# Two order changes at the start of a retention, mixer and MLP kernel: the output decays are loaded ahead of the first chunk's values, and the first chunk's x is finished ahead of its state

## The chip, the cores and the metric

The kernel runs on one core of a Trainium2 chip, in one launch. The metric is the device time of the launch in microseconds (us). The engines are named as in the profile: PE is TensorE (matmul; PEld its weight loads), DVE is VectorE, ACT is ScalarE, POOL is GpSimd, SP is SyncE. Each runs its own stream of instructions in order, and waits for the others only at semaphores. Transfers (DMA) are issued from SP's, ACT's and POOL's queues.

## The reference

Three stages follow each other on two batches of 768 tokens with 512 features (8 heads of 64):

```python
# 1: retention, a decayed running state per head
for t in range(S):
    state = gamma[None, :, None, None] * state + einsum('bhd,bhe->bhde', k[:, :, t], v[:, :, t])
    y[:, :, t] = scale * einsum('bhd,bhde->bhe', q[:, :, t], state)
# 2: x = y as (B, S, 512); a wave-like mixer over tokens, then a channel layer
theta = x @ w_theta
y = einsum('ts,bsd->btd', w_tok_r, x * cos(theta)) + einsum('ts,bsd->btd', w_tok_i, x * sin(theta))
u = x + y
x = u + maximum(u @ w_ch, 0)
# 3: a two-layer mixer over tokens, a two-layer MLP over channels, both with a residual
u = x + (maximum(x^T @ w_tok1, 0) @ w_tok2)^T
out = u + maximum(u @ w_ch1, 0) @ w_ch2
```

The change lies wholly in the first 13 us of stage 1, and only the first of its chunks is touched.

## The kernel before

**Tiling of stage 1.** Each batch's 768 tokens are cut into 6 chunks of 128, so there are 12 chunks, g = 0 to 11. Retention is computed a chunk at a time: the part within the chunk as a masked product of queries and keys, the part from earlier chunks through a state. The decays are constant factors, held in the tile `cst`: the first part (triangle, score, key and carry decays, identity) is loaded by ACT's queue under the semaphore `const_in`, the last part, `out_decay` (C_OUT to N_CONST, 128 x 512 floats, 256 KB), by SP's queue under `decay_in`.

**One chunk's steps**, by the names of the functions and the lines of the profile:

- SP loads q, k (transposed), k and v (by rows) of the chunk into `qkv_in` (L380, 1 MB). Chunk 0 is loaded in two halves: L394 (q and k transposed, semaphore `first_qk_in`) and L395 (k and v by rows, the "values", semaphore `chunk_in[0]`). L396 loads the output decays.
- PE `scores(g)` (L999): queries times keys, 16 matmul records.
- DVE `weigh(g)` (L712): scores times the causal decays, into `prob`.
- PE `outputs(g)` (L1029, from the state, not for the first chunk of a batch; L1039, from `prob` and v), into the banks BK_Y.
- POOL `decay_keys(g)` (L439): k by rows times the key decays, into `k_dec`.
- PE `keys_values(g)` (L1013): the chunk's own contribution to the state, into BK_STATE.
- DVE `advance_state(g)` (L722 for the first chunk of a batch, L725 otherwise): BK_STATE into `state`.
- DVE `finish_x(g)` (L731): BK_Y times `out_decay`, into `res`. This is x of the chunk.
- ACT `x_high(g)` (L553) and DVE `x_low(g)` (L736): x as a pair of rounded parts, for products at higher precision. `theta_high` (ACT, L536) and `theta_low` (DVE, L696, twice) make the same pair of w_theta, once.
- PE `theta(g)` (L982): x times w_theta, 12 matmuls. It waits for `x_lo_ready` and, for the first chunk, `theta_lo`.
- After that come angles, sines and cosines on ACT and DVE, and PE's `turn_x(g)` (L1053).

**What sets the order.** It is written out by hand, engine by engine. PE's order at the start is: two rounds of idle matmuls (L988), scores(0), outputs(0), keys_values(0), scores(1), keys_values(1), outputs(1), theta(0), scores(2), keys_values(2), outputs(2), and so on. DVE's order is: a memset, the causal decays (L809), weigh(0), a wait for `decay_in`, and then for each g advance_state(g), finish_x(g), weigh(g+1), x_low(g); after x_low(0) come the two theta_low. ACT's is x_high(0), then the two theta_high. SP's is the two halves of chunk 0, the output decays, chunk 1, the two halves of w_theta, chunk 2 and so on.

The waits around the change: outputs(1) waits for `x_ready` of finish_x(0), because it writes the banks BK_Y that finish_x(0) reads. keys_values(1) waits for `state_ready` of advance_state(0). SP's load of chunk 3 waits for outputs(0) and keys_values(0) on PE. Nothing else waits for `decay_in` but the DVE.

The quoted functions hold the order of DVE at the start and that of SP's loads.

Of the kernel before, what the change touches and what calls it, by code (L numbers as in the profile page):

```python
# [13 lines left out]
NG = B * NC  # L14
# [72 lines left out]
C_OUT = C_IDENT + P  # L87
N_CONST = C_OUT + DM
# [16 lines left out]
def retention_mixer_mlp(nc, qkv, theta_w, tok, weights, ch2, consts, out):  # L105
    with ExitStack() as ctx:
        def sb(name, shape, dt=F32, within=ctx):
            return within.enter_context(nc.sbuf_tensor(name, shape, dt))

        def sem(name):  # L110
            return ctx.enter_context(nc.semaphore(name))

        cst = sb("cst", [P, N_CONST])
# [108 lines left out]
        def res_half(b, k, half):  # L222
            return res[:, b, k, half * HS:(half + 1) * HS]
# [11 lines left out]
        def parts_of(b, n):  # L235

            return sum(tile in (b, 2) for _, tile in HIDDEN[:n])
# [10 lines left out]
        decay_in = sem("decay_in")  # L248
# [84 lines left out]
        def split_done(eng, i):  # L333
            if i < MIDDLE:
                eng.wait_ge(middle_lo, i + 1)
            else:
                eng.wait_ge(late_lo, i - MIDDLE + 1)
# [35 lines left out]
        @block.sync  # L373
        def _(sp):
            def load_chunk(g):
                if g >= NQ:
                    sp.wait_ge(y_ready, g - NQ + 1)
                if g == NQ:
                    sp.wait_ge(kv_ready, 1)
                sp.dma_start(qkv_in[:, g % NQ, :], qkv[g]).then_inc(chunk_in[g % NQ], 16)  # L380

            def load_piece(i):
                if i >= NSTAGE:
                    split_done(sp, i - NSTAGE)
                sp.dma_start(stage[:, i % NSTAGE, :], weights[i]).then_inc(piece_in[i % NSTAGE], 16)

            def load_third(e):

                q, at = (2, 1, 0)[1 + e // 3], slice(e % 3 * THIRD, (e % 3 + 1) * THIRD)
                if e == 3:  # L390
                    sp.wait_ge(theta_lo, 2)
                sp.dma_start(raw[:, q, at], tok[2 * q, :, at]).then_inc(third_in[e], 16)

            sp.dma_start(qkv_in[:, 0, 0:2 * DM], qkv[0, :, 0:2 * DM]).then_inc(first_qk_in, 16)  # L394
            sp.dma_start(qkv_in[:, 0, 2 * DM:4 * DM], qkv[0, :, 2 * DM:4 * DM]).then_inc(chunk_in[0], 16)  # L395
            sp.dma_start(cst[:, C_OUT:N_CONST], consts[:, C_OUT:N_CONST]).then_inc(decay_in, 16)  # L396
            load_chunk(1)
            for i in range(2):
                at = slice(i * THETA_HALF, (i + 1) * THETA_HALF)
                sp.dma_start(raw[:, 0, at], theta_w[:, at]).then_inc(theta_in[i], 16)  # L400
            for g in range(2, NG):
                load_chunk(g)
                if g < 8:
                    load_third(g - 2)

            sp.wait_ge(zr_ready, NG)
            sp.wait_ge(zi_ready, NG)
            for i in range(N_PIECES):
                load_piece(i)

            split_done(sp, N_PIECES - 1)
            for i in range(2):
                sp.dma_start(w2_raw[:, i, :], ch2[i]).then_inc(w2_in[i], 16)
            for p, r, b in ((1, 0, 0), (4, 1, 0), (5, 1, 1), (6, 0, 1)):
                for i in range(CELLS):
                    m, half = i // 2, i % 2
                    sp.wait_ge(down_kept, p * CELLS + i + 1)
                    sp.dma_start(out[b, 2 * r + m, :, half * HS:(half + 1) * HS],
                                 res_half(b, 2 * r + m, half)).then_inc(out_sent, 16)
            sp.wait_ge(out_sent, 16 * 4 * CELLS)  # L420
# [271 lines left out]
        def _(dve):  # L692
            def theta_low(i):
                at = slice(i * THETA_HALF, (i + 1) * THETA_HALF)
                dve.wait_ge(theta_hi, i + 1)
                dve.scalar_tensor_tensor(out=w_sq[:, 1, at], in0=raw[:, 0, at], scalar=TURNS, in1=f32(w_sq[:, 0, at]),  # L696
                                         op0=ALU.mult, op1=ALU.subtract).then_inc(theta_lo, 1)

            def token_low(p, third):
                at = slice(third * THIRD, (third + 1) * THIRD)  # L700
                dve.wait_ge(tok_hi, 3 * (p if p > 1 else 1 - p) + third + 1)
                dve.tensor_tensor(tw[:, p % 2, 1, at], raw[:, W_RAW[p], at], f32(tw[:, p % 2, 0, at]),  # L702
                                  ALU.subtract).then_inc(tok_lo, 1)
# [6 lines left out]
            def weigh(g):  # L710
                dve.wait_ge(score_ready, g + 1)
                dve.tensor_tensor(prob[:, :, :], ps[:, BK_SCORE:BK_SCORE + 2, :], causal[:, :, :],  # L712
                                  ALU.mult).then_inc(prob_ready, 1)

            def advance_state(g):
                b, c = g // NC, g % NC
                if c == NC - 1:
                    return
                dve.wait_ge(kv_ready, b * (NC - 1) + c + 1)
                new, kv = state[:, (g + 1) % 2, :], ps[:, BK_STATE, 0:H * D // 2]  # L720
                if c == 0:
                    dve.tensor_scalar(new, kv, 1.0, None, ALU.mult).then_inc(state_ready, 1)  # L722
                else:
                    dve.wait_ge(carried_ready, b * (NC - 2) + c)
                    dve.tensor_tensor(new, kv, carried[:, :], ALU.add).then_inc(state_ready, 1)  # L725

            def finish_x(g):
                dve.wait_ge(y_ready, g + 1)
                to = res[:, g // NC, :, g % NC * P:(g % NC + 1) * P].rearrange("p (r m) t -> p r m t", r=2)
                y = ps[:, BK_Y:BK_Y + 2, 0:2 * P].rearrange("p r (m t) -> p r m t", m=2)  # L730
                dve.tensor_tensor(to, y, out_decay.rearrange("p r (m t) -> p r m t", m=2),  # L731
                                  ALU.mult).then_inc(x_ready, 1)

            def x_low(g):
                dve.wait_ge(x_hi_ready, g + 1)
                dve.tensor_tensor(x_lo[:, g % 2, :, :], res[:, g // NC, :, g % NC * P:(g % NC + 1) * P],  # L736
                                  f32(x_hi[:, g % 2, :, :]), ALU.subtract).then_inc(x_lo_ready, 1)

            def reduce_angle(g):
                t = turn[:, g % 2, :]  # L740
                dve.wait_ge(whole_ready, g + 1)
                if g >= 2:
                    dve.wait_ge(zi_ready, g - 1)

                dve.scalar_tensor_tensor(out=t, in0=fold[:, g % 2, :], scalar=-ROUND, in1=bank(BK_THETA + g % 2),
                                         op0=ALU.add, op1=ALU.subtract).then_inc(frac_ready, 1)
                dve.wait_ge(frac_ready, g + 1)
                dve.tensor_scalar(t, t, 0.5, -0.5, ALU.min, ALU.max).then_inc(angle_ready, 1)
# [13 lines left out]
            def z_low(s):  # L762
                p, i = s // NPAIR, s % NPAIR
                dve.wait_ge(z_hi, s + 1)
                what, hi, lo = z[:, Z_KIND[p], i, :], zs[:, s % NZ, 0, :], zs[:, s % NZ, 1, :]
                if Z_SIGN[p] > 0:
                    dve.tensor_tensor(lo, what, f32(hi), ALU.subtract).then_inc(z_lo, 1)
                else:
                    dve.scalar_tensor_tensor(out=lo, in0=what, scalar=-1.0, in1=f32(hi), op0=ALU.mult,
                                             op1=ALU.subtract).then_inc(z_lo, 1)  # L770
# [43 lines left out]
            for g in range(NG + 2):  # L814
                if 0 <= g - 2:
                    reduce_angle(g - 2)
                if g < NG:
                    advance_state(g)
                    finish_x(g)
                if g + 1 < NG:  # L820
                    weigh(g + 1)
                if g < NG:
                    x_low(g)
                if g == 0:
                    for i in range(2):
                        theta_low(i)
                if g >= NG - 1:
                    z_low(g - (NG - 1))
                if g >= 2:
                    turn_parts(g - 2)  # L830
                    if g < 8:
                        token_low(1 - (g - 2) // 3, (g - 2) % 3)
# [450 lines left out]
```

## Time and profile before

| | |
|---|---|
| median of 3 runs | 435.82 us (435.68 to 436.22) |
| the profiled execution | 435.77 us, of which the span from first to last instruction 434.0 us |
| PE busy | 426.8 us, 98% of the span |
| DVE busy | 278.4 us, 64% |
| ACT busy | 158.3 us, 36% |
| POOL busy | 85.3 us, 20% |
| granted TensorE clock | 0.999 of full speed on average |
| the chain that ended last | PE 96%, DVE 2%, DMA 1% of the span |

Busy shares say how much of the span an engine had an instruction in work. The chain that ended last is followed back from the last instruction, at each step to what released it. Every microsecond outside PE in it is a place where PE had to wait. PE is busy in 98% of the span, so all that PE waits for is a few microseconds, most of them in the first 15. A time in a row of the timeline is the start in us from the span's start and then the duration; the end is their sum. On one engine, neighbouring instructions overlap by a little where neither waits.

### The profile page before, as it was taken

The numbers are of one execution on the slowest core, as the hardware profiler recorded it, in microseconds if no ns is written. First come the engines' busy times: TensorE is split into PE (matmuls) and PEld (weight loads), VectorE is DVE, ScalarE is ACT, GpSimd is POOL, SyncE is SP. The second block draws the span as 40 slices with busy tenths as digits, with TensorE's granted clock in tenths as the row PEclk, the third lists the DMA queues.
The fourth block names the chain that finished last, engine by engine and source line by source line (L and its number), as shares of the span: only waits on it lengthen the run. The fifth ranks groups of instructions, "written<-read, shape, count | busy, mean of one in ns | idle before, by whom it ended". The sixth has DMA issues, their size and how long they took to land.

```text
span 434.0 us, 6621 instructions
## 1 busy us (share of the span) xinstructions
PE 426.8 (98%) x2748; PEld 388.3 (89%) x2748; DVE 278.4 (64%) x383; ACT 158.3 (36%) x231; POOL 85.3 (20%) x75
## 2 busy tenths in 40 slices
PE   7999999999999999999999999999999999999997
PEld 4778878899999999999889988888888899999997
DVE  3799998799999995234415304525211599999951
ACT  1364564744455456112214311101202443555500
POOL 1322241000300006980005803303000110000000
PEclk9999999999999999999999999999999999999999
DMA  8975797540594102030000000003000468340121
GB/s 301 419 269 198 253 270 146 103 145 2 157 220 159 48 2 97 2 115 31 0 2 0 2 0 0 2 0 142 5 0 2 72 154 171 113 67 26 54 74 73
DMA packets 10478, 42.25 MB, mean 97 GB/s; under 512 B 1104, under 2 KB 3280, under 8 KB 8656
## 3 DMA queue, kind: packets, MB, share of 16 engines
q1 hardware_dynamic: 7344, 26.74, 16.6%
q0 software_dynamic: 2960, 14.94, 15.6%
q8 instruction: 22, 0.36, 0.4%
q10 hardware_dynamic: 144, 0.14, 0.1%
q14 instruction: 8, 0.07, 0.1%
HBM read 38.68 MB, written 3.15 MB: 96 GB/s over the span
## 4 chain that ended last, share of the span: by engine, by line
PE 96%; DVE 2%; DMA 1%; ACT 0%; issue 0%; ACTq 0%; DVEq 0%
PE ps L982 85%; PE ps L999 3%; PE ps L1039 3%; PE ps L1053 2%; PE ps L1130 1%; PE ps L1013 1%; PE ps L1029 1%; DMA qkv_in<-qkv 1%; DVE prob L712 1%; DVE h_ops_c L906 0%; DVE w_sq L696 0%; ACT h_ops_c L657 0%; DVE x_lo L736 0%; DVE res L731 0%; DVE res L942 0%
## 5 line engine op out<-in xcount | busy, mean ns | idle before, releaser
L982 PE MATMUL ps<-u,ch 128*128 128x512 f32 x432 | 98.1, 389 | 0.0
L982 PEld LDWEIGHTS ps<-u,ch 128*128 128x128 f32 x432 | 81.1, 188 | 16.8
L982 PE MATMUL ps<-tw,zs 128*128 128x384 f32 x504 | 88.1, 335 | 0.0
L982 PEld LDWEIGHTS ps<-tw,zs 128*128 128x128 f32 x504 | 87.3, 188 | 0.1
L982 PE MATMUL ps<-h_ops_c,w 128*128 128x384 f32 x312 | 57.0, 335 | 0.2
L982 PEld LDWEIGHTS ps<-h_ops_c,w 128*128 128x128 f32 x312 | 54.2, 188 | 0.8 <-DVE h_ops_c L906 0.8
L899 DVE SCALAR_TENSOR_TENSOR h_a<-ps,h_a 128x512 f32<-128x512 f32 (+1 forms) x16 | 8.9, 558 | 44.3 <-PE ps L982 26.3
L580 ACT ACTIVATE zs<-z 128x768 fp32r<-128x768 f32 x28 | 23.7, 846 | 37.0 <-PE ps L982 37.0
L982 PE MATMUL ps<-ut,w_sq 128*128 128x384 f32 x192 | 35.5, 338 | 0.0
L982 PEld LDWEIGHTS ps<-ut,w_sq 128*128 128x128 f32 x192 | 33.0, 188 | 0.0
L982 PE MATMUL ps<-w_sq,x_hi 128*128 128x512 f32 x96 | 30.7, 401 | 0.7 <-DVE w_sq L696 0.7
L642 ACT ACTIVATE h_a<-ps 128x512 f32<-128x512 f32 (+1 forms) x16 | 7.9, 491 | 54.2 <-PE ps L982 54.2
L982 PE MATMUL ps<-h_ops_a,w 128*128 128x384 f32 x144 | 27.6, 334 | 0.0
L982 PEld LDWEIGHTS ps<-h_ops_a,w 128*128 128x128 f32 x144 | 25.2, 188 | 0.1
L454 POOL TENSOR_TENSOR ut<-res,ut 128x384 fp32r<-128x384 f32 x16 | 16.6, 1076 | 33.0 <-ACT ut L585 33.0
L460 POOL TENSOR_TENSOR u<-res,u 128x768 fp32r<-128x768 f32 x8 | 14.7, 1843 | 40.2 <-ACT u L636 40.2
L667 ACT ACTIVATE w<-w_raw 128x1536 fp32r<-128x1536 f32 x7 | 10.4, 1486 | 32.0 <-PE ps L982 32.0
L553 ACT ACTIVATE x_hi<-res 128x512 fp32r<-128x512 f32 x12 | 7.6, 633 | 39.2 <-DVE res L731 39.2
L982 PEld LDWEIGHTS ps<-w_sq,x_hi 128*128 128x128 f32 x96 | 17.2, 188 | 4.0 <-issue 0.9
L849 DVE SCALAR_TENSOR_TENSOR res<-ps,res 128x384 f32<-128x384 f32 x16 | 8.9, 558 | 18.3 <-PE ps L982 18.3
L702 DVE TENSOR_TENSOR tw<-raw,tw 128x768 fp32r<-128x768 f32 x21 | 20.7, 984 | 0.0
L626 ACT ACTIVATE u<-ps 128x512 fp32r<-128x512 f32 x12 | 7.2, 600 | 34.2 <-PE ps L1130 34.2
(106 smaller groups left out, 639.0 us busy)
## 6 DMA issues: line engine op xcount, KB each, us to landing
qkv_in<-qkv SPq DMA_DIRECT2D x11, 1024.0 KB, 7.5
raw<-tok POOLq DMA_DIRECT2D x7, 1152.0 KB, 9.0
stage<-weights SPq DMA_DIRECT2D x11, 512.0 KB, 3.4
w_raw<-ch POOLq DMA_DIRECT2D x7, 768.0 KB, 6.8
cols_out<-res SPq DMA_DIRECT2D x16, 192.0 KB, 1.8
raw<-tok SPq DMA_DIRECT2D x6, 384.0 KB, 8.6
w_raw<-ch SPq DMA_DIRECT2D x2, 768.0 KB, 5.3
raw<-tok POOLq DMA_DIRECT2D x3, 384.0 KB, 9.2
```

The costliest lines, as they stand in the source:

```text
L454: pool.tensor_tensor(u_half(1, b, k, half), res_half(b, k, half), f32(u_half(0, b, k, half)), ALU.subtract).then_inc(ut_lo, 1)
L460: pool.tensor_tensor(u[:, b, 1, k, :], res[:, b, k, :], f32(u[:, b, 0, k, :]), ALU.subtract).then_inc(u2_lo, 1)
L580: act.activation(zs[:, s % NZ, 0, :], z[:, Z_KIND[p], i, :], ACT.Copy, scale=Z_SIGN[p]).then_inc(z_hi, 1)
L642: act.activation(hidden_units(f % 2, f // 2, 0)[:, cols], bank(BK_H2[n % 8])[:, 0:cols.stop - cols.start], ACT.Relu).then_inc(h2_first, 1)
L667: act.activation(w2[:, p % 2, 0, :], w2_raw[:, W2_RAW[p], :], ACT.Copy, scale=W2_SIGN[p]).then_inc(w2_hi, 1)
L702: dve.tensor_tensor(tw[:, p % 2, 1, at], raw[:, W_RAW[p], at], f32(tw[:, p % 2, 0, at]), ALU.subtract).then_inc(tok_lo, 1)
L849: dve.scalar_tensor_tensor(out=part, in0=ps[:, BK_M + q % 2, 0:HS], scalar=0.0, in1=part, op0=ALU.max, op1=ALU.add).then_inc(x2_kept, 1)
L899: dve.scalar_tensor_tensor(out=hidden_units(half, phi, 1)[:, cols], in0=bank(BK_H2[n % 8])[:, at:at + cols.stop - cols.start], scalar=0.0, ...
L982: mm = pe.matmul(dst, left(l), right(r), start=first and n == 0, stop=last and n == 2, skip_group_check=True)
L999: mm = pe.matmul(ps[:, BK_SCORE + r, i * P:(i + 1) * P], qkv_in[rows, g % NQ, DM + i * P:DM + (i + 1) * P], qkv_in[rows, g % NQ, i * P:(i ...
L1039: mm = pe.matmul(ps[cols, BK_Y + r, i // 2 * P:(i // 2 + 1) * P], qkv_in[:, g % NQ, 3 * DM + h * D:3 * DM + (h + 1) * D], prob[:, r, i * P ...
L1053: mm = pe.transpose(ps[:, BK_XROW, k * P:(k + 1) * P], res[:, b, k, c * P:(c + 1) * P], ident)
```

## The change

Two things are exchanged. On SP, the load of the output decays (256 KB) is issued ahead of the load of the first chunk's values (512 KB) and no longer behind it. On DVE, for g = 0 alone, finish_x comes ahead of advance_state; for all other chunks the order stays. Nothing is added or removed.

```diff
             sp.dma_start(qkv_in[:, 0, 0:2 * DM], qkv[0, :, 0:2 * DM]).then_inc(first_qk_in, 16)
+            sp.dma_start(cst[:, C_OUT:N_CONST], consts[:, C_OUT:N_CONST]).then_inc(decay_in, 16)
             sp.dma_start(qkv_in[:, 0, 2 * DM:4 * DM], qkv[0, :, 2 * DM:4 * DM]).then_inc(chunk_in[0], 16)
-            sp.dma_start(cst[:, C_OUT:N_CONST], consts[:, C_OUT:N_CONST]).then_inc(decay_in, 16)
             load_chunk(1)
...
             for g in range(NG + 2):
                 if 0 <= g - 2:
                     reduce_angle(g - 2)
-                if g < NG:
+                if g == 0:
+                    finish_x(g)
+                    advance_state(g)
+                elif g < NG:
                     advance_state(g)
                     finish_x(g)
```

SP's queue at the start of the program. The 128x1024 loads are the halves of chunk 0, the 128x512 load is that of the output decays, the 128x2048 load is chunk 1:

```order
 L373 UNCONDITIONAL_BRANCH [waits barrier_Pool_Activation_PE_DVE_SP_release]
 L394 DMA qkv_in<-qkv 128x1024
-L395 DMA qkv_in<-qkv 128x1024
-L396 DMA cst<-consts 128x512
+L395 DMA cst<-consts 128x512
+L396 DMA qkv_in<-qkv 128x1024
 L380 DMA qkv_in<-qkv 128x2048
 L400 DMA raw<-theta_w 128x1024 x2
```

The second and third load have changed places; the first half of chunk 0 still goes first, and chunk 1 and w_theta still come behind all three.

DVE at the start, from the causal decays to x_low(0). L731 is finish_x(0), L722 is advance_state(0), the L712 behind them is weigh(1):

```order
 L809 TENSOR_TENSOR causal<-cst 128x1024 [waits const_in]
 L712 TENSOR_TENSOR prob<-ps,causal 128x1024 [waits score_ready,causal_ready]
-L722 TENSOR_SCALAR state<-ps 128x256 [waits kv_ready,decay_in]
-L731 TENSOR_TENSOR res<-ps,cst 128x4x128 [waits y_ready]
+L731 TENSOR_TENSOR res<-ps,cst 128x4x128 [waits y_ready,decay_in]
+L722 TENSOR_SCALAR state<-ps 128x256 [waits kv_ready]
 L712 TENSOR_TENSOR prob<-ps,causal 128x1024 [waits score_ready]
 L736 TENSOR_TENSOR x_lo<-res,x_hi 128x512 [waits x_hi_ready]
```

finish_x(0) has moved ahead of advance_state(0) and has taken over the wait for the decays. Both still stand between weigh(0) and weigh(1). The orders of PE, ACT and POOL are the same in both kernels.

## Rows read from the trace of the kernel before

**Rows 1.** The page: busy time (share) and instructions.

```profile
PE 426.8 (98%) x2748; PEld 388.3 (89%) x2748; DVE 278.4 (64%) x383; ACT 158.3 (36%) x231; POOL 85.3 (20%) x75
```

**Rows 2.** Chain that ended last, 0 to 15 us: start, duration, what.

```profile
0.74 4.76 DMA qkv_in<-qkv
...
10.24 0.42 DVE state L722
10.66 0.60 DVE res L731
11.26 1.22 DVE prob L712
```

**Rows 3.** Timeline, all engines, 0 to 20 us: start, duration, instruction [idle before <-releaser].

```profile
6.92 1.04 POOL L439 TENSOR_TENSOR k_dec<-qkv_in,cst 128x512 f32<-128x512 f32 x1 [6.47 <-DMA qkv_in<-qkv]
7.28 1.22 DVE L712 TENSOR_TENSOR prob<-ps,causal 128x1024 f32<-128x1024 f32 x1 [0.36 <-PE ps L999]
8.56 1.09 PE L1039 MATMUL ps<-prob,qkv_in 128*64 128x128 f32 x16 [1.40 <-DVE prob L712]
...
9.48 0.63 PE L1013 MATMUL ps<-qkv_in,k_dec 128*64 128x64 f32 x16
9.97 1.04 POOL L439 TENSOR_TENSOR k_dec<-qkv_in,cst 128x512 f32<-128x512 f32 x1 [2.02 <-DMA qkv_in<-qkv]
...
10.05 1.16 PE L999 MATMUL ps<-qkv_in 64*128 64x128 f32 x16
...
10.24 0.42 DVE L722 TENSOR_SCALAR state<-ps 128x256 f32<-128x256 f32 x1 [1.73 <-PE ps L1013]
10.58 0.68 DVE L731 TENSOR_TENSOR res<-ps,cst 128x512 f32<-128x512 f32 x1
...
11.14 0.69 PE L1013 MATMUL ps<-qkv_in,k_dec 128*64 128x64 f32 x16
11.26 1.23 DVE L712 TENSOR_TENSOR prob<-ps,causal 128x1024 f32<-128x1024 f32 x1
11.36 0.63 ACT L553 ACTIVATE x_hi<-res 128x512 fp32r<-128x512 f32 x1 [8.69 <-DVE res L731]
...
11.76 0.67 PE L1029 MATMUL ps<-qkv_in,state 64*64 64x128 f32 x16
11.90 1.99 ACT L536 ACTIVATE w_sq<-raw 128x1024 fp32r<-128x1024 f32 x2
12.40 0.68 DVE L736 TENSOR_TENSOR x_lo<-res,x_hi 128x512 fp32r<-128x512 f32 x1
...
13.00 2.35 DVE L696 SCALAR_TENSOR_TENSOR w_sq<-raw,w_sq 128x1024 fp32r<-128x1024 f32 x2
...
14.36 0.70 PE L982 MATMUL ps<-w_sq,x_hi 128*128 128x512 f32 x2 [0.73 <-DVE w_sq L696]
...
17.30 1.16 PE L999 MATMUL ps<-qkv_in 64*128 64x128 f32 x16
...
18.51 1.23 DVE L712 TENSOR_TENSOR prob<-ps,causal 128x1024 f32<-128x1024 f32 x1 [0.56 <-PE ps L999]
```

**Rows 4.** Timeline, DVE, 22 to 24 us: the same pair of steps for chunk 2.

```profile
22.43 0.68 DVE L731 TENSOR_TENSOR res<-ps,cst 128x512 f32<-128x512 f32 x1
...
23.03 1.22 DVE L712 TENSOR_TENSOR prob<-ps,causal 128x1024 f32<-128x1024 f32 x1
```

**Rows 5.** Timeline, SP's queue, 0 to 3 us: when the loads are issued.

```profile
1.18 0.43 SPq L395 DMA_DIRECT2D qkv_in<-qkv  x1
1.66 0.42 SPq L396 DMA_DIRECT2D cst<-consts  x1
2.12 0.72 SPq L380 DMA_DIRECT2D qkv_in<-qkv  x1
```

**Rows 6.** One line of the code, L395: the load of the values.

```profile
DMA to landing us min/median/max: 5.6/5.6/5.6
```

**Rows 7.** One line of the code, L396: the load of the output decays.

```profile
DMA to landing us min/median/max: 5.8/5.8/5.8
```

**Rows 8.** One line of the code, L380, 0 to 3 us: chunk 1.

```profile
DMA to landing us min/median/max: 7.8/7.8/7.8
```

**Rows 9.** Busy time by stretch: start:end, length, engines, PEclk, DMA share, GB/s.

```profile
0.00:5.50 5.50, 3.78 (x4) 1.17 (x4) 0.48 (x1) 1.49 (x2) 0.20 (x4) 1.00 0.61 184
5.50:10.00 4.50, 3.05 (x48) 2.84 (x48) 2.45 (x2) 0.00 (x0) 1.06 (x2) 1.00 1.02 422
```

## The prediction

> **What bounds the kernel now.** I read the page first: PE is busy in 98% of the span [rows 1], so a change elsewhere counts only where PE waits for it. Then the chain of waits, cut to the first 15 us, because the change touches nothing later. The reader is to see there that DVE's advance_state(0) and finish_x(0) both stand in it, directly ahead of weigh(1) [rows 2]. That looks like a place where taking finish_x early would pay. A chain names one releaser for each step, though, so the third view is the timeline of the same stretch, to see how late a second releaser was [rows 3]. Last come the loads: when they are issued [rows 5] and how long they take to land [rows 6 to 8].
>
> What PE waits for in this stretch: theta(0) starts at 14.36 after 0.73 us of idleness, released by the first theta_low on DVE. DVE reaches that by weigh(1) from 11.26, x_low(0) from 12.40, theta_low from 13.00 [rows 3]. So the question of the whole change is: does weigh(1), x_low(0) or the first theta_low start earlier?
>
> **DVE's exchange, step by step.** outputs(0) runs on PE from 8.56 for 1.09, to 9.65. keys_values(0) ends at 9.48 + 0.63 = 10.11, and advance_state(0) begins 0.13 later, at 10.24 [rows 3]. In the new order finish_x(0) waits for outputs(0) alone. With the same 0.13 it starts at about 9.78 instead of 10.58, 0.80 earlier, and ends at 9.78 + 0.68 = 10.46. advance_state(0) follows with the usual overlap of 0.08 (10.24 + 0.42 = 10.66, yet finish_x started at 10.58): it starts at 10.38 and ends at 10.80, 0.14 later than now. DVE could then begin weigh(1) at 10.80 - 0.08 = 10.72.
>
> Could it do so before? finish_x(0) ended at 10.58 + 0.68 = 11.26 and weigh(1) started at 11.26, with no overlap at all. Where weigh follows finish_x and its scores are long done, it starts 23.03 - 22.43 = 0.60 behind it, 0.08 before its end [rows 4]. So DVE was free for weigh(1) at 11.18 and still began at 11.26. What it waited for then is scores(1), which PE ran from 10.05 for 1.16, to 11.21; 0.05 later weigh(1) began. The same pair at chunk 2, where the profile names PE as releaser: scores(2) ends at 17.30 + 1.16 = 18.46, weigh(2) starts at 18.51, again 0.05 later [rows 3]. DVE and PE came to weigh(1) within 0.08 us of each other. The chain names finish_x because it was in work until then, but the gate is scores(1).
>
> scores(1) itself follows keys_values(0) on PE without idleness (10.11, and the next starts at 10.05, overlapped), and that follows outputs(0), which follows weigh(0), which the change doesn't touch. So weigh(1) stays at 11.26: gain 0.00. The 0.54 us that DVE gains (11.26 - 10.72) turn into idleness in front of weigh(1).
>
> x_low(0) needs weigh(1) off the engine (12.40) and x_high(0). x_high(0) ended at 11.36 + 0.63 = 11.99 and now ends 0.80 earlier, but it wasn't what x_low(0) waited for: gain 0.00. The first theta_low starts at 13.00, while the first theta_high ends at 11.90 + 1.99/2 + 0.04 (half the overlap of the pair) = 12.94, and x_low(0) ends at 13.08 with 0.08 of overlap. Both allow 13.00; only theta_high can move earlier: gain 0.00. theta(0) stays at 14.36.
>
> **The step made later.** advance_state(0) ends 0.14 later, at 10.80. keys_values(1), which waits for it, starts at 11.14 because scores(1) is ahead of it: 0.34 us of cover. outputs(1) starts at 11.76 and waits for finish_x(0), which is now early. Cost 0.00; if the cover were gone, the 0.73 us that PE idles before theta(0) would still take it up. POOL's next step that reads the state stands behind the key decays of chunk 2 and isn't moved. SP's load of chunk 3 waits for PE alone.
>
> **SP's exchange, step by step.** Landings now: values 1.18 + 5.6 = 6.8, output decays 1.66 + 5.8 = 7.5, chunk 1 at 2.12 + 7.8 = 9.9 [rows 5 to 8]. q and k of chunk 0 land at 0.74 + 4.76 = 5.50 [rows 2]. Issue order and landing order agree, and the engines are full from 5.50 to 10.00, at 422 GB/s [rows 9]. So 256 KB (0.262 MB) put ahead of the values cost them 0.262 / 422 = 0.62 us: they land at 7.4 and the decays by about 6.2. The swap of two loads of one queue leaves the bytes ahead of chunk 1 the same, and two issues of 0.43 and 0.42 remain two such issues: chunk 1 still lands at 9.9.
>
> Who waits for the values: POOL's key decays of chunk 0, started 6.92, now at about 7.54, ending at 8.58; PE asks for them at 9.48, so 0.90 us are left. outputs(0) asks for the values at 8.56: 1.1 us are left. Cost 0.00. Who waits for the output decays: only DVE, at 9.78 in the new order. They were there at 7.5, 2.3 us before even the new place of finish_x(0) asks. Moving their load brings 0.00: the exchange on DVE doesn't need it. The two key decays on POOL took 1.04 each, one under weigh(0), one under advance_state(0) and finish_x(0) [rows 3], so the neighbours on DVE don't set their length.
>
> **The costs that no row shows.** The first is chunk 1's landing after an exchange of the loads ahead of it. Its margin is narrow: landed at 9.9, used by POOL at 9.97 and by PE at 10.05, so about 0.1 us. Lower bound: the landing stays or comes earlier, 0.00, since PE is busy until 10.11 anyway. Upper bound: chunk 1 pays for the decays' 0.262 MB once more, 0.62 us, of which 0.62 - 0.1 = 0.52 reach PE. I take 0.00, because equal bytes at a full rate are the nearest row. The second is the landing of the first q and k, with which all begins. By 5.50 the engines had moved 184 x 5.50 = 1.01 MB [rows 9], while those two and ACT's constants (139 KB) are 0.67 MB; so 0.34 MB of later loads had gone through beside them. Now the load next in line is 0.262 MB, and the values behind it fill the rest. Bounds: at best the difference of 0.08 MB stays out, 0.08 / 422 = 0.2 us earlier; at worst as much later. I take 0.00.
>
> The Trainium skill has a rule that speaks against the exchange: "DMA: Bandwidth & Descriptors", section "Two DMAs through the same engine are not ordered", says that on one queue descriptors start in order but nothing orders DMAs across the 16 engines, so an order of issue doesn't fix an order of landing. By that rule the landing of chunk 1 could come out later than equal bytes say, which is the second rival below; by the rows the three landings are in order and the sum stays 0.00. No row here shows an order that broke.
>
> **Sum.** 0.00 (weigh(1)) + 0.00 (theta) + 0.00 (state later) + 0.00 (loads) = 0. The profiled execution took 435.77 us, 0.05 below the median of 435.82, so the prediction is 435.8 us. What a measurement of this kernel can tell from no change is about 0.2%, 0.87 us.
>
> **Rivals.**
>
> 1. The chain is right and finish_x(0) was the gate: the 0.80 us by which it moves reach theta(0), giving 435.8 - 0.8 = 435.0. For it: the chain names it [rows 2], and ACT's wait of 8.69 us for it ends 0.80 earlier. Against it: scores(1) ends at 11.21 and keys_values(1) starts on PE only at 11.14 [rows 3], so scores(1) could not have been done much sooner than the row says. Even if ends on PE are off by 0.1, this gives 0.1. Chance 4%.
> 2. The slower side: chunk 1 lands too late. The place is scores(1) on PE; it decides from a landing after about 10.0, and each further microsecond goes through weigh(1) and x_low(0) to theta(0) in full, since that chain has no slack. At the upper bound above it is 435.8 + 0.5 = 436.3. To cost over 0.87 us, chunk 1 would have to land 1.0 us later, longer than 0.62 for the whole of the decays. Chance 8%, half of it above 0.87 us.
> 3. The values arrive too late for keys_values(0), because they now stand behind the decays. It decides from a landing 0.90 us later than I expect, at 8.3; if the values' landing took chunk 1's 7.8 us from its new issue at about 1.6, that is 9.4, and PE's wait is 1.1: 436.9. Against it: it would need three times the 0.62 us of the bytes. Chance 2%.
> 4. The first q and k land up to 0.2 us earlier: 435.6. Chance 6%, within 0.2% of no change.
>
> **How the numbers follow.** My forecast has 80%. Faster by over 0.2%: only rival 1 with a disturbance in its favour, and what I overlook, 4%. Slower by over 0.2%: half of rival 2, rival 3 at 1.1, together with the overlooked, 6%. The same: 90%. The runs before spread over 435.68 to 436.22. The range takes these in, below it reaches to rival 1 and above to rival 2: 435.0 to 436.4.
>
> **What would show it.** L731 at about 9.8 and L722 after it at about 10.4 on DVE, then about 0.5 us of idleness released by PE's L999, and weigh(1) again at about 11.26: right. weigh(1) clearly before 11.2 would show that scores(1) wasn't the gate. POOL's first key decays at about 7.5 and the second at 9.97 show the loads right; a second one later than 10.05, with PE idle before scores(1), would be rival 2. x_high(0) on ACT at about 10.55 and theta(0) still at 14.36, with 0.7 us of idleness before it, would show that the early x wasn't needed. The prediction is wrong if theta(0) starts more than 0.9 us away from 14.36, counted from the landing of the first q and k, or if anything behind it differs, where I expect the same trace to the end.

## The result and the profile after

The changed kernel takes 439.24 us (median of 18 runs, 435.86 to 439.94) against 435.92 us for the kernel before in the same sessions (18 runs, 435.45 to 437.56). The ratio is 1.0049, 95% interval 1.0033 to 1.0065: slower, by about half a percent. The prediction said no change.

The runs don't scatter, they fall into groups. With the mean granted TensorE clock that each run lists:

| | F: about 436, clock 0.999 or 1.0 | M: about 437.5, clock 0.995 or 0.996 | S: 438.3 to 440, clock 0.999 or 1.0 |
|---|---|---|---|
| before, the 116 runs beside the experiments | 84 | 32 | 0 |
| changed, 18 runs | 3 | 5 | 10 |

So the half percent isn't a delay that every run has: three runs of the changed kernel are as fast as those of the kernel before. It is the share of the groups that changed, and 10 of 18 runs are in one that the kernel before shows in none of 116.

The profiled execution of the changed kernel took 439.23 us (span 437.4 us) and is one of group S. Its chain that ended last (start, duration, what), to be read against [rows 2]:

```profile
0.74 4.96 DMA qkv_in<-qkv
...
5.75 2.10 PE ps L1002 x16
...
7.95 1.24 DVE prob L712
...
9.23 1.97 PE ps L1042 x16
11.20 0.85 PE ps L1016 x16
12.06 1.67 PE ps L1002 x16
...
13.75 1.23 DVE prob L712
14.98 0.60 DVE x_lo L736
15.57 1.99 DVE w_sq L696
```

The code's lines behind 817 moved by 3: L1002 is scores, L1042 outputs, L1016 keys_values, L985 theta. DVE's advance_state and finish_x are gone from the chain. In this execution that says nothing of the new order: PE is so late with scores(1) that they are gone from the chain of `before_less160` (below) too, which has the old order on DVE. PE's part has grown: outputs(0) took 1.09 us in [rows 3] and takes 1.97 here.

The same stretch in the timeline of the changed kernel:

```profile
5.75 2.08 PE L1002 MATMUL ps<-qkv_in 64*128 64x128 f32 x16 [0.50 <-DMA qkv_in<-qkv]
...
11.32 0.69 DVE L731 TENSOR_TENSOR res<-ps,cst 128x512 f32<-128x512 f32 x1 [2.15 <-PE ps L1042]
...
12.11 0.42 DVE L722 TENSOR_SCALAR state<-ps 128x256 f32<-128x256 f32 x1
...
13.63 0.69 PE L1016 MATMUL ps<-qkv_in,k_dec 128*64 128x64 f32 x16
13.75 1.23 DVE L712 TENSOR_TENSOR prob<-ps,causal 128x1024 f32<-128x1024 f32 x1 [1.22 <-PE ps L1002]
...
15.10 1.37 POOL L439 TENSOR_TENSOR k_dec<-qkv_in,cst 128x512 f32<-128x512 f32 x1 [3.92 <-DMA qkv_in<-qkv]
15.49 3.62 DVE L696 SCALAR_TENSOR_TENSOR w_sq<-raw,w_sq 128x1024 fp32r<-128x1024 f32 x2
...
17.70 0.70 PE L985 MATMUL ps<-w_sq,x_hi 128*128 128x512 f32 x2 [1.58 <-DVE w_sq L696]
```

The step that all waits for, theta(0), starts at 17.70 and not at 14.36 [rows 3]: 3.34 us later. The terms, each from the starts of two rows:

- q and k land at 5.70 and not 5.50, scores(0) starts 0.20 later.
- weigh(0) starts at 7.95 and not 7.28: 0.47 more, because scores(0) takes 2.08 us and not 1.61.
- weigh(1) starts at 13.75 and not 11.26: 1.82 more, because outputs(0), keys_values(0) and scores(1) are slow too.
- from weigh(1) to theta_low it is 1.74 us in both.
- theta_low to theta(0) is 2.21 and not 1.36: 0.85 more.

They add up to 3.34. The two spans differ by 437.4 - 434.0 = 3.4, so nothing of weight happens later.

Why are PE's instructions slow? One line of the code in one stretch, scores(0), first in the kernel before, 5 to 8 us (min/median/max in ns):

```profile
L999 PE MATMUL ps<-qkv_in x16: 271/313/578, 5.5 to 6.9; 64*128 64x128 f32 x16
```

then in the changed kernel, the same stretch, and behind it scores(1), 11.9 to 14 us:

```profile
L1002 PE MATMUL ps<-qkv_in x16: 417/418/579, 5.7 to 7.4; 64*128 64x128 f32 x16
...
L1002 PE MATMUL ps<-qkv_in x16: 271/389/579, 12.0 to 13.4; 64*128 64x128 f32 x16
```

The shortest record is 271 ns or 417 ns, the engine at one of two rates. In the kernel before PE goes over to the fast rate within scores(0): the first records of under 417 ns start at 6.35 us, those of 271 at 6.55. In the changed kernel no record of scores(0) is fast, outputs(0) and keys_values(0) are slow throughout, and the fast rate comes in the second half of scores(1): the first records of under 417 ns start at 13.00 us, those of 271 at 13.20. (The expectations below say 6.3 and 12.8 for these two places, which is too early.)

That is TensorE's clock, though the page's row of granted clock shows full speed in both kernels even here. A trace in which the clock falls settles which level is which, that of `loads_only` (below), whose profiled run is of group M. Its busy time by stretch (start:end, length, engines, PEclk, DMA share, GB/s):

```profile
8.50:9.00 0.50, 0.50 (x10) 0.50 (x10) 0.00 (x0) 0.00 (x0) 0.22 (x1) 0.82 0.97 410
9.00:12.00 3.00, 3.00 (x38) 2.88 (x36) 1.02 (x2) 0.00 (x0) 1.04 (x1) 0.50 1.04 426
13.00:14.00 1.00, 0.88 (x26) 0.57 (x22) 1.00 (x2) 1.00 (x2) 0.00 (x0) 1.00 0.99 417
```

From 9 to 12 us the granted clock is 0.50, 1.2 of 2.4 GHz. Its scores(0) and its scores(1), 10.6 to 12.5 us:

```profile
L999 PE MATMUL ps<-qkv_in x16: 272/272/373, 5.6 to 6.5; 64*128 64x128 f32 x16
...
L999 PE MATMUL ps<-qkv_in x16: 271/417/579, 10.7 to 12.3; 64*128 64x128 f32 x16
```

So 417 ns is the record at 1.2 GHz, and 272 the one at 2.4 GHz. This is what a run of group M looks like: the clock is already full at scores(0), PE then idles 1.5 us until weigh(0) is done, and the clock falls at about 8.8 us. In the profiled run of group S the clock hasn't risen yet, and doesn't until scores(1). The granted clock that is listed leaves out a clock that has not yet risen, which is why group S lists 1.0. Runs without a trace are put into their group by time and listed clock alone.

### The profile page after: what moved, and what is told of

It reads as the page before. It is cut to its first block, busy times and chain, and to the rows that moved or that the text cites. A ratio compares the mean times of both kernels' runs of the same rounds, so it can differ in the third digit from the quotient of the medians.

```text
span 437.4 us, 6621 instructions
## 1 busy us (share of the span) xinstructions
PE 429.2 (98%) x2748; PEld 390.3 (89%) x2748; DVE 279.4 (64%) x383; ACT 158.8 (36%) x231; POOL 86.9 (20%) x75
## 4 chain that ended last, share of the span: by engine, by line
PE 96%; DVE 2%; DMA 1%; ACT 0%; issue 0%; ACTq 0%; DVEq 0%
PE ps L985 85%; PE ps L1002 3%; PE ps L1042 3%; PE ps L1056 2%; PE ps L1133 1%; PE ps L1016 1%; DMA qkv_in<-qkv 1%; PE ps L1032 1%; DVE prob L712 1%; DVE w_sq L696 0%; DVE h_ops_c L909 0%; ACT h_ops_c L657 0%; DVE x_lo L736 0%; DVE res L945 0%; ACTq L654 0%
## 5 line engine op out<-in xcount | busy, mean ns | idle before, releaser
L985 PE MATMUL ps<-u,ch 128*128 128x512 f32 x432 | 98.1, 389 | 0.0
L985 PEld LDWEIGHTS ps<-u,ch 128*128 128x128 f32 x432 | 81.1, 188 | 16.8
L985 PE MATMUL ps<-tw,zs 128*128 128x384 f32 x504 | 88.1, 335 | 0.0
L985 PEld LDWEIGHTS ps<-tw,zs 128*128 128x128 f32 x504 | 87.4, 188 | 0.1
L985 PE MATMUL ps<-h_ops_c,w 128*128 128x384 f32 x312 | 57.0, 335 | 0.2
L985 PEld LDWEIGHTS ps<-h_ops_c,w 128*128 128x128 f32 x312 | 54.2, 188 | 0.8 <-DVE h_ops_c L909 0.8
L985 PE MATMUL ps<-ut,w_sq 128*128 128x384 f32 x192 | 35.5, 338 | 0.0
L985 PEld LDWEIGHTS ps<-ut,w_sq 128*128 128x128 f32 x192 | 33.0, 188 | 0.0
L985 PE MATMUL ps<-w_sq,x_hi 128*128 128x512 f32 x96 | 30.8, 402 | 1.6 <-DVE w_sq L696 1.6
L985 PE MATMUL ps<-h_ops_a,w 128*128 128x384 f32 x144 | 27.6, 334 | 0.0
L985 PEld LDWEIGHTS ps<-h_ops_a,w 128*128 128x128 f32 x144 | 25.2, 188 | 0.1
L985 PEld LDWEIGHTS ps<-w_sq,x_hi 128*128 128x128 f32 x96 | 17.1, 188 | 5.1 <-issue 1.8
```

Source lines behind the costliest of these rows:

```text
L985: mm = pe.matmul(dst, left(l), right(r), start=first and n == 0, stop=last and n == 2, skip_group_check=True)
```

## The experiments

Each ratio is to runs of the kernel before in the same session. There were four sessions, each on a chip of its own. "F/M/S" counts runs in the groups above; there are 12 of each kernel, and 6 of `own_tensor`. Two runs, one each of `after_mid` and `own_values`, took 2.4 ms and stand in no group. The one of `after_mid` was the profiled one: its landing stands in the table, but nothing below rests on its trace. In `split_values` the three runs under M have that clock (0.996) at 436.6 to 436.8 us.

| kernel | median us | ratio to before, 95% interval | F/M/S | q, k landing, us from issue |
|---|---|---|---|---|
| before_mid | 435.52 | 0.9984 (0.9971 to 0.9996) | 12/0/0 | 4.5 |
| before_plus64_mid | 435.57 | 0.9989 (0.9978 to 1.0001) | 12/0/0 | 4.5 |
| late_decays_mid | 435.58 | 0.9997 (0.9987 to 1.0007) | 12/0/0 | 4.5 |
| dve_only | 435.68 | 0.9994 (0.9975 to 1.0013) | 10/1/1 | 4.5 |
| after_plus64_mid | 435.93 | 1.0002 (0.9992 to 1.0012) | 12/0/0 | 5.1 |
| after_mid | 436.02 | 1.0006 (0.9991 to 1.0022) | 8/0/3 | 5.0 |
| after_plus64 | 436.13 | 1.0008 (0.9991 to 1.0025) | 8/4/0 | 5.0 |
| split_values | 436.28 | 1.0007 (0.9996 to 1.0018) | 9/3/0 | 4.3 |
| before_less64 | 436.47 | 0.9998 (0.9979 to 1.0016) | 6/6/0 | 4.5 |
| own_values | 437.69 | 1.0038 (1.0019 to 1.0058) | 3/5/3 | 4.9 |
| loads_only | 437.80 | 1.0044 (1.0025 to 1.0063) | 1/6/5 | 4.9 |
| before_less160 | 438.89 | 1.0050 (1.0031 to 1.0070) | 1/2/9 | 4.8 |
| own_tensor | 439.36 | 1.0069 (1.0049 to 1.0089) | 0/2/4 | 5.1 |

**Which half of the change?** `loads_only` has the first hunk of the change alone, `dve_only` the second:

```diff
+            sp.dma_start(cst[:, C_OUT:N_CONST], consts[:, C_OUT:N_CONST]).then_inc(decay_in, 16)   # loads_only
             sp.dma_start(qkv_in[:, 0, 2 * DM:4 * DM], qkv[0, :, 2 * DM:4 * DM]).then_inc(chunk_in[0], 16)
-            sp.dma_start(cst[:, C_OUT:N_CONST], consts[:, C_OUT:N_CONST]).then_inc(decay_in, 16)
...
+                if g == 0:                # dve_only
+                    finish_x(g)
+                    advance_state(g)
```

> The exchange of the two loads alone; DVE's order as before. Theory A (the loads): in the changed kernel the first q and k landed 0.2 us later, PE idled 0.50 us and not 0.31 us ahead of scores(0), and its matmuls then stayed at the slow durations (417 ns a record) until about 12.8 us, where before they changed to 271 ns at about 6.3 us. If so, this kernel is like the changed one: about 439 us in most runs, weigh(1) at about 13.7 us in its trace. Theory B (DVE's exchange is the cause): this kernel is like the one before, about 435.9 us, weigh(1) at 11.3 us.

> The exchange of finish_x(0) and advance_state(0) on DVE alone; the loads in the order of before. Theory A: like the kernel before, 435.9 us in most runs, with the first q and k at 5.5 us, the matmuls at 271 ns from about 6.3 us, weigh(1) at 11.26 us and about 0.5 us of idleness on DVE ahead of it. Theory B: about 439 us.

Measured: 437.80 us and 435.68 us, 1.0044 and 0.9994. The loads do it all, the exchange on DVE nothing that can be told. Theory A had `loads_only` at 439 us in most runs: 5 of 12 are there, and 6 are in group M, among them the profiled one, in which weigh(1) starts at 12.62. The trace of `dve_only` shows the step on DVE as the prediction worked it out. Its timeline:

```profile
9.69 0.69 DVE L731 TENSOR_TENSOR res<-ps,cst 128x512 f32<-128x512 f32 x1 [1.26 <-PE ps L1042]
...
9.96 1.16 PE L1002 MATMUL ps<-qkv_in 64*128 64x128 f32 x16
...
10.29 0.41 DVE L722 TENSOR_SCALAR state<-ps 128x256 f32<-128x256 f32 x1
10.48 0.63 ACT L553 ACTIVATE x_hi<-res 128x512 fp32r<-128x512 f32 x1 [7.80 <-DVE res L731]
...
11.17 1.23 DVE L712 TENSOR_TENSOR prob<-ps,causal 128x1024 f32<-128x1024 f32 x1 [0.47 <-PE ps L1002]
```

x of the first chunk is finished early, and weigh(1) still begins 0.05 us behind scores(1) (9.96 + 1.16 = 11.12), after 0.47 us of idleness that PE releases. One of its 12 runs is of group S, which the 116 of the kernel before don't have; one run is too few to say more.

**Is it the loads, or PE's idleness behind them?** Both kernels leave the loads as they were in their parent and change only idle matmuls.

```diff
             pe.wait_ge(idle_ready, 1)
-            keep_warm(2, DM)          # before_less64, from the kernel before
+            keep_warm(1, DM)
+            keep_warm(1, DM - 64)
...
             keep_warm(2, DM)          # after_plus64, from the changed kernel
+            keep_warm(1, 64)
```

> The changed kernel with one idle matmul more, of 64 columns, behind the two of 512 (by the 1.9 us of one of 512 at the slow rate it takes about 0.24 us). Landings as in the changed kernel, but PE's idleness ahead of scores(0) is 0.50 - 0.24 = 0.26 us, a little less than the 0.31 us of before. Theory A1 (what counts is how long PE idled before scores(0)): back to about 435.9 to 436.1 us in most runs. Theory A2 (the later landing or the loads themselves count, not PE's idleness): stays at about 439 us.

> The kernel before with the second idle matmul 64 columns shorter (0.24 us less). The loads and their landing are those of before (5.5 us), but PE idles 0.31 + 0.24 = 0.55 us ahead of scores(0). Theory A1 (PE's idleness counts): most runs at about 439 us, with slow matmuls until about 12.8 us. Theory A2 (the loads count): 435.9 us as before.

`after_plus64`: 436.13 us, and no run of group S, where its parent has 10 of 18. q and k landed as late as in the parent (5.0 us), yet PE idled 0.25 us ahead of scores(0):

```profile
5.81 1.62 PE L1002 MATMUL ps<-qkv_in 64*128 64x128 f32 x16 [0.25 <-DMA qkv_in<-qkv]
8.83 1.09 PE L1042 MATMUL ps<-prob,qkv_in 128*64 128x128 f32 x16 [1.41 <-DVE prob L712]
```

outputs(0) is back at 1.09 us. `before_less64` was a miss for A1 as put: no run of group S, and M in 6 of 12. In its profiled execution q and k landed so early (4.5) that PE idled only 0.29 us: the edit was smaller than the scatter of the landing. So a larger one was made, with `keep_warm(1, DM - 160)` as the second:

> The kernel before, loads untouched, with the second idle matmul 160 columns shorter (about 0.60 us less at the slow rate): PE idles about 0.6 to 0.9 us ahead of scores(0), more than in the changed kernel (0.50 us), at the landing of before (4.5 to 4.8 us after the issue). Theory A1 (PE's idleness counts): the times of 439 us appear, which the kernel before has in none of 35 runs and the changed one in 10 of 18; median 437.5 to 439. Theory A2 (only the loads count): two groups as before, 435.6 and 437.4 us, none at 439.

438.89 us, 9 of 12 runs of group S, with the loads of the kernel before. Its timeline of PE:

```profile
5.53 2.08 PE L999 MATMUL ps<-qkv_in 64*128 64x128 f32 x16 [0.83 <-DMA qkv_in<-qkv]
9.02 1.97 PE L1039 MATMUL ps<-prob,qkv_in 128*64 128x128 f32 x16 [1.40 <-DVE prob L712]
10.78 1.07 PE L1013 MATMUL ps<-qkv_in,k_dec 128*64 128x64 f32 x16
```

These are the durations of the changed kernel. More idleness ahead of scores(0) brings its slow group without the change, less takes it away with the change. That settles the cause: the exchange of the loads costs time through PE's clock. These edits change both how long PE idles ahead of scores(0) and how much it has worked before; the exchange itself changes only the first, since the idle matmuls take 3.78 us in both kernels.

**The middle group.** The kernel `after_mid` puts work under PE's wait for weigh(0):

```diff
             scores(0)
+            keep_warm(1, 384)
```

`before_mid` is the kernel before with that line. The two kernels with `plus64_mid` in their name have it and, ahead of scores(0), the `keep_warm(1, 64)` of `after_plus64`.

> The changed kernel with one idle matmul of 384 columns between scores(0) and outputs(0), where PE waits 1.4 us for weigh(0) (0.7 us of work at the full rate, 1.4 us at the slow one). Theory M: the middle group of runs (437.4 to 438.2 us, mean granted clock 0.995 to 0.996) is one in which the clock was already full at scores(0) and fell after that wait. Then this kernel has no middle group: 3 of 18 at 435.9 become about half, at 435.7 to 436.2, and the group at 439.3 stays, since it is decided ahead of scores(0). Rival: the middle group comes from a fall later in the kernel, then the groups stay as they are.

> The changed kernel with both: one idle matmul of 64 columns ahead of scores(0) and one of 384 columns behind it. Theory A1 and M together: nearly all runs in the fastest group, 435.7 to 436.2 us, median about 436.0, no run at 437.4 or more. If the idle matmuls don't decide it, the groups at 437.7 and 439.3 stay.

`after_mid`: no run has a clock under 0.999, so M is gone, as theory M says. The other half of that expectation fell: the slowest group didn't stay at 439.3 but went to 437.4 to 437.6 (3 of 11 runs; they are counted under S, since the clock has the mark of it). It may be that the idle matmuls behind scores(0) also help a clock that missed its first rise; no trace of such a run was taken, so this isn't shown. With both (`after_plus64_mid`) all 12 runs lie in 435.78 to 436.37 us.

> The kernel before with one idle matmul of 384 columns between scores(0) and outputs(0). The kernel before has two groups of runs, 435.4 to 436.3 us at a mean clock of 0.999 or more, and 436.8 to 437.9 us at 0.995 or 0.996. Theory M (the clock is already full at scores(0) and falls after the wait of 1.4 us for weigh(0)): no run at 0.996 or less, none over 436.5, median about 435.6. Rival: the second group comes from elsewhere and stays at about 3 in 10 runs.

> The kernel before with both idle matmuls, 64 columns ahead of scores(0) and 384 behind it. Theory: as before_mid, all runs in one group; the 64 columns end at about 5.5 us, later than q and k land in many runs (5.2 to 5.5), so the median is the same or up to 0.2 us above that of before_mid. Beside the changed kernel with the same two (435.93 us) it shows what the exchange itself costs once the clock no longer decides: equal if it costs nothing, about 0.3 us if the later landing of q and k goes through.

Both as expected, 12 of 12 runs in group F. `before_mid` is faster than the kernel before, 0.9984 (0.9971 to 0.9996), by 0.16%. Between the two kernels with both idle matmuls there remain 435.93 - 435.57 = 0.36 us. As an estimate that is what the exchange costs once the clock no longer decides; it is from two chips, and the intervals of the two ratios, 1.0002 and 0.9989, overlap, so it isn't shown clear of noise. In their profiled executions scores(0) starts at 5.85 and at 5.49 us, also 0.36 apart.

**Why do q and k land later?** They are first in the queue in all kernels. Three kernels change only what stands behind them:

```diff
-            sp.dma_start(qkv_in[:, 0, 2 * DM:4 * DM], qkv[0, :, 2 * DM:4 * DM]).then_inc(chunk_in[0], 16)
+            sp.dma_start(qkv_in[:, 0, 2 * DM:3 * DM], qkv[0, :, 2 * DM:3 * DM]).then_inc(first_key_in, 16)   # split_values
+            sp.dma_start(qkv_in[:, 0, 3 * DM:4 * DM], qkv[0, :, 3 * DM:4 * DM]).then_inc(chunk_in[0], 16)
...
+            sp.dma_start(cst[:, C_OUT:N_CONST], decays).then_inc(decay_in, 16)               # own_tensor
             sp.dma_start(qkv_in[:, 0, 2 * DM:4 * DM], qkv[0, :, 2 * DM:4 * DM]).then_inc(chunk_in[0], 16)
-            sp.dma_start(cst[:, C_OUT:N_CONST], consts[:, C_OUT:N_CONST]).then_inc(decay_in, 16)
...
-            sp.dma_start(qkv_in[:, 0, 2 * DM:4 * DM], qkv[0, :, 2 * DM:4 * DM]).then_inc(chunk_in[0], 16)
+            sp.dma_start(qkv_in[:, 0, 2 * DM:4 * DM], values).then_inc(chunk_in[0], 16)      # own_values
```

`decays` and `values` are tensors with the same numbers, in rows of their own.

> The kernel before with the values' load (512 KB, 4 KB a row) split into two of 256 KB (2 KB a row), the keys' rows first, the output decays still behind both. Asks why q and k of chunk 0 land later in the changed kernel (4.9 to 5.0 us after their issue against 4.5 to 4.8). Theory L1 (a 256 KB load directly behind them does it, whatever it holds): landing at 4.9 to 5.0 us and times at 439 us in some runs, median over 437. Theory L2 (it is the decays' tensor, or chance): landing at 4.5 to 4.8 us, median about 435.9.

> The exchange of the two loads alone, with the output decays read from a tensor of their own (rows of 2048 bytes, contiguous) and not from the back part of the rows of 3160 bytes from which ACT's queue reads the other constants at the same time. Theory L3 (the way in which these rows lie in memory delays q and k of chunk 0): landing back at 4.3 to 4.8 us after the issue, median about 435.9 and no runs at 439. Theory L4 (it is the place in the queue, not the source): landing 4.9 to 5.1, groups as in the kernel with the loads exchanged (436.2, 437.7, 439.3 us).

L1 fell, and so did L3. In `split_values` a 256 KB load stands right behind q and k, and they land earlier than anywhere (4.3 us). Its 436.28 us, above the 435.9 of L2, fit chunk 1, which is now issued fifth and lands at 10.48 us: PE idles 0.32 us for it ahead of scores(1), which starts at 10.53. In `own_tensor` the decays' rows are contiguous and nobody else reads them, and q and k land at 5.1. What was left is what the next load shares with q and k: the values lie in the same rows of the same tensor.

> The kernel before, its order of loads and its sizes, with the values of chunk 0 (512 KB, 4 KB a row) read from a tensor of their own and not from the rows in which q and k of chunk 0 also lie. Theory N1 (a next load out of the same rows lets q and k land early): landing 4.9 us or more after the issue, and times of 439 us in some runs, median over 437. Theory N2 (it is the decays' place, whatever the tensor): landing 4.3 to 4.8, groups as before (435.6 and 437.4), none at 439.

The runs fit N1: only the source of the values differs from the kernel before, the landing is 4.9 us, and 3 of 11 runs are of group S, against none of 17 of the kernel before beside them. Leaving out `after_mid`, q and k land 4.3 to 4.8 us after the issue in the eight kernels whose next load reads the same rows, and 4.9 to 5.1 in the six where it reads another tensor. It is one execution each, the two ranges lie 0.1 us apart, and a new input may also have moved the others in memory. Whether the same rows are needed or the same tensor will do was not tried, and why the memory serves them so isn't shown by any trace here.

**The opposite of the change.** `late_decays_mid` is `before_mid` with the output decays' load moved behind chunk 1's:

```diff
-            sp.dma_start(cst[:, C_OUT:N_CONST], consts[:, C_OUT:N_CONST]).then_inc(decay_in, 16)
             load_chunk(1)
+            sp.dma_start(cst[:, C_OUT:N_CONST], consts[:, C_OUT:N_CONST]).then_inc(decay_in, 16)
```

> The kernel before with the idle matmul of 384 columns behind scores(0), and the output decays loaded behind chunk 1, the opposite of the change. Chunk 1 then lands 0.6 us earlier (about 9.3 us), the decays at about 10 us. Theory (chunk 1's landing is close to being the gate of scores(1)): 0 to 0.3 us faster than before_mid, since PE is busy with chunk 0 until about 10. Rival: the decays become the gate of the state and x of chunk 0 on DVE, 0 to 0.3 us slower.

435.58 us against 435.52 for `before_mid`: the same. Chunk 1 landed 0.5 us earlier (9.1 against 9.6), and scores(1) started at 9.44 and not at 9.69. The rival's step is in the trace too: advance_state(0) waited for the decays until 9.79, though keys_values(0) was done at 9.51, and weigh(1) started at 10.73, 0.13 us behind scores(1). theta(0) was 0.10 us earlier all the same (13.90 against 14.00), but in the profiled execution chunk 2 came late and POOL's key decays for it started at 16.21 and not at 14.83. Whether that late landing is the rule or a single event stays open.

## Why the prediction was wrong

**DVE's exchange: right.** Its steps hold to 0.1 us in `dve_only`: finish_x(0) at 9.69 (9.78 predicted, and outputs(0) started 0.09 earlier there, at 8.47), 0.47 us of idleness ahead of weigh(1) (0.54), x_high(0) early and not waited for. The ratio is 0.9994 with one inside the interval. Rival 1, the chain's own reading, is refuted by it: finish_x(0) started 0.89 us earlier and weigh(1) only 0.09, as much as outputs(0). The chain had named finish_x because it ended within 0.08 us of scores(1).

**The loads: the step that failed is the landing of q and k, in its size and, above all, in its price.** "I take 0.00" stands there with bounds of 0.2 us to both sides. The profiled landing came 0.20 us later, the upper bound; in the other kernels with the exchange it is 0.1 to 0.3 later than in [rows 2]. [rows 2] is itself one execution and a late one: in five of the other seven kernels whose next load reads the same rows the landing is 4.5 us after the issue, not 4.8, so the usual delay is rather 0.4 to 0.6 us, as an estimate. The prediction took any such delay as a shift of the whole program, 0.2 us for 0.2 us. That was the mistake. The landing also sets how long PE idles ahead of scores(0), 0.31 us in the kernel before and 0.50 in the changed one, and with that whether PE's clock rises in scores(0) (at about 6.5 us) or only in scores(1) (at about 13.1). Where it is the second, as in 10 of 18 runs, 0.20 us of delay become 3.4.

**A rival that was missing.** None of the four had PE's rate in it. Two signs were in the trace of before. Within one group of identical records the durations ran from 271 to 578 ns, which [rows 3] hide, since a timeline row gives only the sum (1.61 us for scores(0), against 1.16 for scores(1) with the same 16 records). And the program has idle matmuls ahead of scores(0), in a function named `keep_warm`: work without a result ahead of a wait is there for the clock, so whatever moves the end of that wait has to be priced at both rates. The price is outputs(0), keys_values(0) and scores(1) once at each rate. By the rows of the changed kernel it is 1.97 - 1.09 = 0.88 us for outputs(0) alone.

**Rival 2** named the right side with the wrong mechanism. It looked for the lateness at chunk 1. The landings kept the order of issue (5.7, 6.4, 7.7 and 10.1 us). Chunk 1 landed at 2.12 + 8.0 = 10.1, after the point of 10.0 from which I let it decide, but PE was still in outputs(0) then. **Rival 3** didn't happen: the values landed at 1.65 + 6.0 = 7.7, 0.3 later than worked out, and keys_values(0) followed outputs(0) without a wait. **Rival 4** guessed at the landing with the wrong sign.

**The term behind it that nobody asked for.** 0.85 of the 3.34 us are theta_low on DVE. The two take, in the changed kernel from 15 to 20 us:

```profile
L696 DVE SCALAR_TENSOR_TENSOR w_sq<-raw,w_sq x2: 1630/1848/2066, 15.5 to 17.5; 128x1024 fp32r<-128x1024 f32 x2
```

In the kernel before each took 1.22 us. The first took 2.07 here; it started at 15.49, while POOL's key decays of chunk 2 ran from 15.10 to 16.47. A lateness of 2.5 us brought it under a POOL instruction that it had been ahead of. The Trainium skill, "SBUF — State Buffer", section "Who interferes with whom", says that a VectorE instruction with two SBUF inputs contends with a GpSimd one that reads SBUF, and that the later one waits for the first to finish. The trace agrees: 16.47 - 15.49 = 0.98 us of overlap, 0.85 us of extra length. I had concluded from two key decays of 1.04 us that DVE and POOL don't meet; those lay under instructions with one input from PSUM.

**The range** of 435.0 to 436.4 rested on the spread of three runs, 435.68 to 436.22, and took it for that of the kernel. 32 of the 116 runs beside the experiments are of group M: three runs didn't show a group that more than a quarter of all runs belong to. The chance of 6% for slower had no term for that.

## What to carry to other kernels

- Where a program keeps TensorE busy with idle matmuls until its first data land, the wait behind them has a price other than its length. Look at min and max of identical records around it, and price what follows at both rates before anything is moved in the queue that feeds it. Idle work under the second wait (here 384 columns behind scores(0)) took the scatter of 2 us away in the old order of loads, 12 of 12 runs in the fastest group; in the new order it left 3 of 11 slower, and took 64 columns ahead of scores(0) as well.
- A chain of waits names one releaser. Whether removing it pays is read from the second one: compare its end with the start of the waiting instruction, and look for the small overlap that neighbours have where neither waits.
- If runs fall into groups, count the groups before comparing medians, and take more than three runs for the baseline.

## What the runs showed of the hardware

- TensorE's rate in the first 13 us went with how long the engine had idled ahead of scores(0). Of 14 profiled executions, four (`before_mid`, `late_decays_mid`, `after_plus64_mid`, `loads_only`) had the fast rate from the first record of scores(0), so that idleness decided nothing in them. In seven the rate rose in scores(0) or, in `split_values`, between it and outputs(0): the idleness was up to 0.31 us in six and 0.46 in `own_values`. In three it was 0.50, 0.60 and 0.83 us, and the rate rose only in scores(1) or behind it. The same kernel falls into different groups from run to run, so that length isn't all; what else decides was not tried. The Trainium skill, "TensorE: Matmul & The Clock Gate", section "Part 1: The HAM clock gate (the "warmup" mystery)", says that the throttled rate is the default and activity releases it, and that the transition point varies from run to run. The runs agree: up to scores(0) PE's instructions are the same in `before` and `before_mid`, and the first has its slow rate, 417 ns a record, still in scores(0), while the last idle matmul of the second took 657 ns and not 1057.
- The granted clock that a profile lists showed only a clock that fell later, as in `loads_only` (0.50 from 9 to 12 us). In group S it says 1.00 while records take 417 ns and not 271.
- The first load in SP's queue, the same 512 KB in all kernels, landed 4.3 to 4.8 us after its issue where the next one read the same rows of the same tensor (eight profiled executions), and 4.9 to 5.1 us where it read another tensor (six).
- A VectorE instruction with both inputs in SBUF took 2.07 us and not 1.22 when it started 0.98 us before the end of a GpSimd one that reads SBUF (theta_low in the changed kernel).
